# A routed mixture kernel: where the third routing's values are read back, a second PSUM bank, and new places for the routing passes

## The chip, the cores and the metric

One core of one Trainium2 chip. The time is that of one execution on the device, in microseconds (us). The engines are TensorE (PE in the profile: matmuls; its weight loads are PEld), VectorE (DVE), ScalarE (ACT), GpSimd (POOL) and SyncE (SP, which here only starts transfers).

## The reference

Three stages, one after the other. `x` has 1792 rows of 768. The second stage has 8 experts, each of which takes 224 tokens; who goes where is decided by a greedy walk over all logits in falling order.

```python
# 1. sigmoid attention, 4 x 12 heads, 448 tokens, head size 64
scores = scale * np.matmul(q, k.transpose(0, 1, 3, 2)) - np.log(S)
x = np.matmul(1.0 / (1.0 + np.exp(-scores)), v)        # -> (1792, 768)
# 2. routed experts: each token to one expert, each expert full at 224
logits = x @ w_gate
for idx in np.argsort(-logits.flatten()):
    tok, e = idx // E, idx % E
    if assigned[tok] >= 0 or counts[e] >= cap: continue
    assigned[tok] = e; counts[e] += 1
h = np.maximum(x[mask] @ w1[e], 0.0); out[mask] = h @ w2[e]
# 3. a common network with PReLU, d_ff = 2048
h = x @ w_in
g = np.maximum(h, 0.0) + alpha * np.minimum(h, 0.0)
return g @ w_out
```

## The kernel before

**The routed part.** The greedy walk is done as eight routings (r = 0 to 7; "the third" is r = 2). Each finds, for the experts still open, the threshold of the 224th largest value, picks the one expert that is settled by it and its tokens, and closes both. `rank(r)` finds the threshold in eight **passes**: in each, VectorE compares all values (`rank_in`, 128 x 1792) with a trial value and counts the hits, then a few tiny operations make the next trial. For that each expert's 1792 values must stand on 16 partitions. From the third routing on they get there through DRAM: `store_suit` writes `suit` to `suit_flat` (56 KB), `spread_suit` reads it back 16 times over into `rank_in` (896 KB). Both are issued by GpSimd, in one queue with its gathers. `fill(r)` then makes the flags of the tokens, their places and their indices, in three parts between which TensorE does small sums (`spread_thr`, `sum_flags`, `sum_idx`), and the next values.

**The big products.** Every product is made of three float32r matmuls (high x high, high x low, low x high); the high part is a rounding by ScalarE and the low part a subtraction by VectorE. A weight chunk so prepared is a **unit**, in a ring of 12 slots. TensorE walks through steps, one unit each, 60 to a pair of experts: the first expert's w1 (steps 0 to 5, `hidden`, L902), its w2 (6 to 13, `returned`, L932), the second expert's w1 (14 to 19) and w2 (20 to 27), then the common network of both for 448 columns (28 to 59): `ffn_in(m)` (L955) at 28, 29, 31, 33 ... makes one of 16 pieces of h, and `ffn_out(m)` (L967) at 30, 32, 34 ... adds its product with w_out into six banks (`OUT_BANK + d`, banks 1 to 6). There are four pairs (`q`, 0 to 3). w1 and w2 chunks are gathered by GpSimd (L567, L575), since the expert is known only when the kernel runs; SyncE loads the common network's units from DRAM (L511), each once its slot is free.

**Between two steps of the common network** ScalarE empties bank 0 (`above`, `below`, L1151 and L1152) and counts `in_taken`; VectorE makes PReLU of it (`below`, L1464); ScalarE rounds it (`g_high`); VectorE makes `g_low` (L1469), and only then can `ffn_out` begin. All `ffn_in` write bank 0.

**What sets the order.** All engines walk the same steps. VectorE's function `go(s)` issues its work of all steps up to s: `y_low` at steps 14 and 28, `h_low` (L1450) at 6 and 20, PReLU, `g_low`, the low parts of the gathered tokens (`x_low`, L1433) and of the weight units up to seven steps ahead (L1441). A table says at which step each routing pass stands: `PASS_AT[r]` for the eight passes, and then the steps of threshold, flags, indices (`THR_AT`, `FLAGS_AT`, `IDX_AT`) and of the six pieces in which the gathered tokens are turned (`SEL_AT`). A pass at step s is issued after `go(s)`, and whatever belongs to step s + 1 stands behind it. VectorE works in order, so a pass delays it all by some 3 us.

## Time and profile before

| | us |
|---|---|
| median of 3 runs | 1041.22 (1040.79 to 1042.23) |
| the profiled execution's own time | 1040.79 |
| its span in the trace | 1039.1 |
| TensorE busy | 998.8 (96%) |
| VectorE, ScalarE, GpSimd busy | 572.7 (55%), 389.3 (37%), 188.0 (18%) |
| granted TensorE clock, mean | 0.992 |

The span is the trace from the first to the last instruction. A busy TensorE says that matmuls were under way, not that they ran at full speed; the clock column (1.00 is 2.4 GHz, 0.50 is 1.2 GHz) tells the latter. Rows of the trace name an instruction by its line, and what ended the idle time before it.

### The profile page before, as it was taken

How to read it: one execution, taken by the hardware profiler on the slowest of the kernel's cores; microseconds unless marked ns; L12 is line 12 of the kernel's file. 1: busy time of each engine (PE TensorE's matmuls, PEld its weight loads, DVE VectorE, ACT ScalarE, POOL GpSimd, SP SyncE). 2: the span in 40 equal slices, each digit the busy share in tenths (PEclk: the TensorE clock that was granted, in tenths of full speed). 3: DMA queues.
4: the chain of work that ended last, by engine and by line, in shares of the span. 5: the costliest groups of instructions: out<-in, count | busy, mean ns of one | idle time of the engine just before them, and what ended most of it. 6: DMA issues, size and time to landing. Idle time of an engine off the chain costs nothing.

```text
span 1039.1 us, 16704 instructions
## 1 busy us (share of the span) xinstructions
PE 998.8 (96%) x6533; PEld 857.1 (82%) x6533; DVE 572.7 (55%) x1299; ACT 389.3 (37%) x625; POOL 188.0 (18%) x202
## 2 busy tenths in 40 slices
PE   8999999988979999999999999999999999999997
PEld 5555555557978898799989998998999999989996
DVE  4444444598655827947953685496439537221112
ACT  5676676401341124356322224542222356122212
POOL 0010100105520011243301015350100335100001
PEclk9999999999989999999999999999999999999999
DMA  9999996407488685866877855679696436976601
GB/s 210 271 274 273 256 287 198 175 21 249 152 278 277 209 224 181 282 142 214 290 282 234 252 172 122 202 217 377 212 237 213 158 113 193 337 263 215 215 27 54
DMA packets 121476, 222.34 MB, mean 214 GB/s; under 512 B 51424, under 2 KB 69216, under 8 KB 121408
## 3 DMA queue, kind: packets, MB, share of 16 engines
q1 hardware_dynamic: 87152, 120.11, 37.3%
q0 software_dynamic: 21280, 91.59, 28.4%
q10 hardware_dynamic: 12976, 9.70, 3.9%
q8 instruction: 47, 0.77, 0.3%
q14 instruction: 21, 0.17, 0.0%
HBM read 184.84 MB, written 36.52 MB: 213 GB/s over the span
## 4 chain that ended last, share of the span: by engine, by line
PE 85%; DVE 9%; issue 2%; ACT 2%; DMA 1%; POOLq 0%; POOL 0%; DVEq 0%; ACTq 0%
PE psum L955 20%; PE psum L967 19%; PE psum L932 11%; PE psum L902 11%; PE psum L694 8%; PE psum L678 7%; DVE hits L1541 4%; PE psum L897 2%; PE psum L662 2%; PE psum L705 1%; PE psum L927 1%; DMA stage<-x_rows,tok_idx 1%; DVE unit L1441 1%; PE psum L849 1%; PE psum L713 1%
## 5 line engine op out<-in xcount | busy, mean ns | idle before, releaser
L955 PE MATMUL psum<-y_high,unit 128*128 128x448 f32 x768 | 230.9, 368 | 4.4 <-ACT below L1152 4.3
L967 PE MATMUL psum<-g_high,unit 128*128 128x448 f32 x756 | 227.8, 369 | 4.3 <-DVE g_low L1469 4.2
L955 PEld LDWEIGHTS psum<-y_high,unit 128*128 128x128 f32 x768 | 144.2, 188 | 17.9 <-ACT below L1152 5.8
L967 PEld LDWEIGHTS psum<-g_high,unit 128*128 128x128 f32 x756 | 142.0, 188 | 18.9 <-DVE g_low L1469 7.8
L955 PE MATMUL psum<-y_low,unit 128*128 128x448 f32 x384 | 140.3, 365 | 0.0
L1441 DVE TENSOR_TENSOR unit<-raw,unit 128x768 fp32r<-128x768 f32 (+1 forms) x106 | 109.9, 1059 | 51.5 <-ACT unit L1125 44.8
L967 PE MATMUL psum<-g_low,unit 128*128 128x448 f32 x378 | 138.2, 366 | 0.0
L1151 ACT ACTIVATE above<-psum 128x448 f32<-128x448 f32 x64 | 34.9, 545 | 248.8 <-PE psum L955 248.8
L932 PE MATMUL psum<-h_high,unit 128*128 128x224 f32 x672 | 118.5, 280 | 8.8 <-issue 8.8
L1464 DVE SCALAR_TENSOR_TENSOR below<-below,neg_alpha,above 128x448 f32<-128x448 f32 x64 | 43.8, 684 | 147.0 <-ACT below L1152 146.8
L902 PE MATMUL psum<-x_high,unit 128*128 128x224 f32 x672 | 117.3, 276 | 0.0
L932 PEld LDWEIGHTS psum<-h_high,unit 128*128 128x128 f32 x672 | 105.5, 196 | 9.4 <-issue 9.3
L1062 ACT ACTIVATE probs<-psum,gate_bias 112x896 f32<-112x896 f32 x96 | 91.5, 1004 | 55.7 <-PE psum L678 55.7
L1125 ACT CAST unit<-raw 128x768 fp32r<-128x768 f32 (+1 forms) x106 | 93.7, 923 | 29.6 <-DMA raw<-in_moe_w_dram,w_idx 29.2
L902 PEld LDWEIGHTS psum<-x_high,unit 128*128 128x128 f32 x672 | 103.7, 192 | 0.1
L1541 DVE TENSOR_SCALAR_CACHE_REDUCE hits<-rank_in,trial 128x1792 bf16<-128x1792 f32 x49 | 101.6, 2073 | 0.0
L932 PE MATMUL psum<-h_low,unit 128*128 128x224 f32 x336 | 93.4, 278 | 0.0
L567 POOL DMA_INDIRECT raw<-in_moe_w_dram,w_idx x48 | 48.9, 1019 | 245.8 <-PE psum L967 142.6
L902 PE MATMUL psum<-x_low,unit 128*128 128x224 f32 x336 | 92.1, 274 | 0.0
L575 POOL DMA_INDIRECT raw<-in_moe_w_dram,w_idx x64 | 71.9, 1123 | 70.5 <-PE psum L902 20.7
L694 PE MATMUL psum<-probs,v_in 112*64 112x448 f32 x384 | 82.5, 551 | 0.0
L955 PEld LDWEIGHTS psum<-y_low,unit 128*128 128x128 f32 x384 | 72.2, 188 | 5.5
(184 smaller groups left out, 1319.4 us busy)
## 6 DMA issues: line engine op xcount, KB each, us to landing
unit<-ffn_parts SPq DMA_DIRECT2D x120, 768.0 KB, 6.7
ffn_parts<-pre_parts POOLq DMA_DIRECT2D x24, 768.0 KB, 6.7
ffn_parts<-unit SPq DMA_DIRECT2D x8, 768.0 KB, 5.5
q_in<-in_q_dram SPq DMA_DIRECT2D x24, 224.0 KB, 5.5
v_in<-in_v_dram SPq DMA_DIRECT2D x24, 224.0 KB, 7.5
x_rows<-x_tok POOLq DMA_DIRECT2D x8, 672.0 KB, 5.9
rank_in<-suit_flat POOLq DMA_DIRECT2D x6, 896.0 KB
k_in<-in_k_dram SPq DMA_DIRECT2D x23, 224.0 KB, 7.0
```

What stands on the lines that cost most here:

```text
L567: pool.indirect_dma_start(out=raw[:, u % UNIT_RING, LOW, :], out_offset=None, in_=w1_rows, in_offset=at(w1_idx[:, r % IDX_RING, c:c + 1])) ...
L575: pool.indirect_dma_start(out=raw[:, u % UNIT_RING, LOW, 0:D], out_offset=None, in_=w2_rows, in_offset=at(w2_idx[:, r % IDX_RING, c:c + 1] ...
L678: last = pe.matmul(psum[0:P, 2 * h + c, 0:S], k_part[hp % 2][rows, j * P:(j + 1) * P], q_part[hp % 2][rows, :], start=(i == 0), stop=(i == 2))
L694: last = pe.matmul(O[DH * h:DH * h + DH, 0:S], v_in[hp % V_RING][:, h, kj, :], probs[hp % 2][:, h, kj, :], start=(kj == 0), stop=(kj == JT ...
L902: last = pe.matmul(to, w, x[r % 2][:, c, :], start=(opens and i == 0), stop=(closes and i == 2), skip_group_check=True)
L932: last = pe.matmul(to, w, h[:, c, :], start=(opens and i == 0), stop=(closes and i == 2), skip_group_check=True)
L955: last = pe.matmul(psum[:, IN_BANK, 0:PAIR], w, y[:, c, :], start=(c == 0 and i == 0), stop=(c == DC - 1 and i == 2))
L967: last = pe.matmul(psum[:, OUT_BANK + d, 0:PAIR], w, g[:, m % 2, :], start=(m == 0 and i == 0), stop=(m == (FC - 1 if q < GROUPS - 1 else ...
L1062: act.activation(probs[hp % 2][:, h, 2 * step:2 * step + 2, :], psum[0:P, 2 * h:2 * h + 2, 0:S], ACT.Sigmoid, bias=gate_bias[:], scale=flo ...
L1125: act.copy(unit[:, u % UNIT_RING, HIGH, 0:width(u)], raw[:, u % UNIT_RING, LOW, 0:width(u)]).then_inc(w_rounded, 1)
L1441: dve.tensor_tensor(unit[:, u % UNIT_RING, LOW, 0:width(u)], raw[:, u % UNIT_RING, LOW, 0:width(u)], unit[:, u % UNIT_RING, HIGH, 0:width( ...
L1541: then(dve.tensor_scalar(marks, values, limit[:].bitcast(F32), None, ALU.is_ge, ALU.add, accum_out=counts[:]))
```

## The change

1. The third routing's store and read are taken from GpSimd's queue and put into SyncE's, ahead of the common network's loads: the store when the values are made, the read when the store has landed and the second expert's tokens are gathered. VectorE's first pass of r = 2 waits for a semaphore of their own.
2. `ffn_in(1)` writes bank 6, the last of the six of the result, instead of bank 0, and no longer waits for bank 0 to be emptied. `ffn_out(0)` waits, before its last product (the one that opens bank 6), for ScalarE to have emptied it.
3. In later even routings two gathers stand between store and read.
4. The passes of r = 2, r = 3 and of the even routings r = 4 and 6 stand at other steps.

```diff
+        def in_bank(m):
+            return OUT_BANK + DC - 1 if m == 1 else IN_BANK
...
                 if r == 2:
-                    passes, later = (21, 22, 23, 29, 30, 31, 32, 33), (34, 35, 37, 41)
+                    passes, later = (21, 22, 23, 24, 29, 30, 31, 32), (33, 34, 36, 40)
                 elif r == 3:
-                    passes, later = range(45, 53), (54, 55, 57, STEPS + 5)
+                    passes, later = (42, 43, 44, 46, 48, 50, 51, 52), (54, 55, 57, STEPS + 5)
                 elif r % 2 == 0:
-                    passes, later = (9, 11, 13, 16, 22, 24, 28, 29), (31, 32, 34, 38)
+                    passes, later = (9, 11, 13, 16, 18, 21, 23, 25), (31, 32, 34, 38)
...
+            sp.wait_ge(suit_done, 3)
+            sp.dma_start(suit_flat[0].rearrange("e (p g) -> p e g", g=G), suit[:]).then_inc(third_stored, 16)
+            sp.wait_ge(third_stored, 16)
+            for t in range(TILES):
+                sp.wait_ge(first_gathered[t], 32)
+            sp.dma_start(rank_in[:], suit_flat[0].unsqueeze(1).to_broadcast([E, DIGIT, P * G])).then_inc(third_loaded, 16)
             for duo in range(GROUPS):
                 for u in range(STEPS * duo + 2 * OWN, STEPS * duo + STEPS):
...
-            store_suit(2)
-            gather_w2(1, range(3))
-            spread_suit(2)
-            gather_w2(1, range(3, EC))
+            gather_w2(1)
...
                     if q < GROUPS - 2:
-                        repeat_suit(2 * q + 4)
-                    gather_w2(2 * q + 2, range(early, EC))
+                        store_suit(2 * q + 4)
+                    gather_w2(2 * q + 2, range(early, min(early + 2, EC)))
+                    if q < GROUPS - 2:
+                        spread_suit(2 * q + 4)
+                    gather_w2(2 * q + 2, range(early + 2, EC))
...
             def ffn_in(q, m):
                 u = in_unit(q, m)
                 routing(u)
-                if m > 0:
+                if m > 1:
                     pe.wait_ge(in_taken, FC * q + m)
...
-                        last = pe.matmul(psum[:, IN_BANK, 0:PAIR], w, y[:, c, :],
+                        last = pe.matmul(psum[:, in_bank(m), 0:PAIR], w, y[:, c, :],
...
+                    if m == 0 and d == DC - 1:
+                        pe.wait_ge(in_taken, FC * q + 2)
...
-                        dve.wait_ge(rank_loaded, 16 * (r - 1))
+                        if r == 2:
+                            dve.wait_ge(third_loaded, 16)
+                        else:
+                            dve.wait_ge(rank_loaded, 16 * (r - 2))
```

What stands in GpSimd's row around the second expert's gathers: before, the third routing's store (`suit_flat`) and read (`rank_in`) among the gathers of w1 (128 x 1024) and w2 (128 x 768), ...

```order
L584 DMA stage<-x_rows,tok_idx 112x768 x2
L567 DMA raw<-in_moe_w_dram,w_idx 128x1024 x3
L607 DMA suit_flat<-suit 112x8x16
L575 DMA raw<-in_moe_w_dram,w_idx 128x768 x3
L611 DMA rank_in<-suit_flat 128x1x1792
L575 DMA raw<-in_moe_w_dram,w_idx 128x768 x5
```

... and now, in the same row, followed by the next pair's tokens and the fourth routing's store and read:

```order
L598 DMA stage<-x_rows,tok_idx 112x768 x2
L581 DMA raw<-in_moe_w_dram,w_idx 128x1024 x3
L589 DMA raw<-in_moe_w_dram,w_idx 128x768 x8
L598 DMA stage<-x_rows,tok_idx 112x768 x2
L621 DMA suit_flat<-suit 112x8x16
L625 DMA rank_in<-suit_flat 128x1x1792
```

The two have gone to SyncE, and the eight w2 gathers are one run.

VectorE's row in the second and the third pair, from the fourth pass of r = 4 and 6 to the low part of h (`hits` begins a pass, and the four rows with it are its rest; `unit` is the split of weight chunks), before:

```order
L1541 TENSOR_SCALAR hits,counts<-rank_in,trial 128x1792
L1542 STREAM_TRANSPOSE spread<-counts 128x32
L1544 SCALAR_TENSOR_TENSOR spread_own,digit<-spread,by_digit 128x32
L1558 TENSOR_TENSOR trial<-digit,base 128x1
L1561 TENSOR_TENSOR base<-trial,next_bits 128x1
L1441 TENSOR_TENSOR unit<-raw,unit 128x768 x3
L1450 SCALAR_TENSOR_TENSOR h_low<-psum,h_high 128x448 x4
L1441 TENSOR_TENSOR unit<-raw,unit 128x768 x2
```

And now, from the end of the fourth pass:

```order
L1580 TENSOR_TENSOR base<-trial,next_bits 128x1
L1457 TENSOR_TENSOR unit<-raw,unit 128x768 x2
L1560 TENSOR_SCALAR hits,counts<-rank_in,trial 128x1792
L1561 STREAM_TRANSPOSE spread<-counts 128x32
L1563 SCALAR_TENSOR_TENSOR spread_own,digit<-spread,by_digit 128x32
L1577 TENSOR_TENSOR trial<-digit,base 128x1
L1580 TENSOR_TENSOR base<-trial,next_bits 128x1
L1457 TENSOR_TENSOR unit<-raw,unit 128x768
L1466 SCALAR_TENSOR_TENSOR h_low<-psum,h_high 128x448 x4
L1457 TENSOR_TENSOR unit<-raw,unit 128x768 x2
```

The fifth pass stands between the second and the third split, ahead of the low part of h.

VectorE's row in the first pair, around the low part of y, now (before, the pass rows that stand first here came behind `y_low` and `below`):

```order
L1560 TENSOR_SCALAR hits,counts<-rank_in,trial 128x1792
L1561 STREAM_TRANSPOSE spread<-counts 128x32
L1563 SCALAR_TENSOR_TENSOR spread_own,digit<-spread,by_digit 128x32
L1577 TENSOR_TENSOR trial<-digit,base 128x1
L1580 TENSOR_TENSOR base<-trial,next_bits 128x1
L1474 TENSOR_TENSOR y_low<-psum,y_high 128x2x224 x3
L1480 SCALAR_TENSOR_TENSOR below<-below,neg_alpha,above 128x448
L1560 TENSOR_SCALAR hits,counts<-rank_in,trial 128x1792
```

One more pass (the fourth) stands ahead of `y_low`; behind `below` follows a pass as before, now the fifth.

## Rows read from the trace of the kernel before

**Rows 1.** The page, part 1: busy us, share of the span, instructions

```profile
PE 998.8 (96%) x6533; PEld 857.1 (82%) x6533; DVE 572.7 (55%) x1299; ACT 389.3 (37%) x625; POOL 188.0 (18%) x202
```

**Rows 2.** Waits (total, times, longest), then the chain (start, us, what)

```profile
PE psum L932 <- issue: 8.8, 3, 7.4
...
300.08 7.38 issue
307.47 19.19 PE psum L932 x144
...
492.94 16.08 PE psum L902 x144
510.21 16.31 PE psum L932 x144
```

**Rows 3.** Timelines of ScalarE and VectorE: start, us, instruction [idle before, releaser]

```profile
305.01 0.83 ACT L1125 CAST unit<-raw 128x768 fp32r<-128x768 f32 x1 [0.82 <-DMA raw<-in_moe_w_dram,w_idx]
...
306.75 2.21 DVE L1450 SCALAR_TENSOR_TENSOR h_low<-psum,h_high 128x448 fp32r<-128x448 f32 x4
...
325.92 1.97 DVE L1458 TENSOR_TENSOR y_low<-psum,y_high 128x448 fp32r<-128x448 f32 x3 [5.43 <-ACT y_high L1146]
```

**Rows 4.** Table by stretches: busy of each engine, clock, DMA share, GB/s

```profile
281.00:290.00 9.00, 9.00 (x74) 8.98 (x75) 7.93 (x11) 7.49 (x12) 6.59 (x7) 1.00 0.91 307
290.00:293.00 3.00, 3.00 (x30) 3.00 (x28) 2.72 (x3) 1.61 (x2) 2.39 (x3) 1.00 0.49 151
293.00:303.30 10.30, 7.08 (x64) 6.90 (x62) 0.66 (x1) 0.83 (x1) 2.75 (x3) 1.00 0.99 294
303.30:307.40 4.10, 0.00 (x0) 0.00 (x0) 2.78 (x5) 3.22 (x6) 0.00 (x0) 0.50 1.03 401
307.40:313.40 6.00, 5.93 (x28) 5.96 (x29) 5.90 (x12) 1.64 (x3) 0.00 (x0) 0.50 0.47 159
```

**Rows 5.** Timelines of GpSimd, SyncE and TensorE around the read

```profile
288.24 0.68 POOL L611 DMA_DIRECT2D rank_in<-suit_flat  x1 [1.19 <-DMA suit_flat<-suit]
289.22 1.64 POOL L575 DMA_INDIRECT raw<-in_moe_w_dram,w_idx  x1 [0.30 <-issue]
...
292.15 39.00 SPq L511 DMA_DIRECT2D unit<-ffn_parts  x13
...
280.93 0.80 PE L791 MATMUL psum<-ident,stage 112*128 112x112 f32 x6 [0.76 <-DMA stage<-x_rows,tok_idx]
```

**Rows 6.** Timeline of VectorE ahead of h_low, second and third pair

```profile
504.02 2.07 DVE L1541 TENSOR_SCALAR_CACHE_REDUCE hits<-rank_in,trial 128x1792 bf16<-128x1792 f32 x1
...
506.89 2.69 DVE L1441 TENSOR_TENSOR unit<-raw,unit 128x768 fp32r<-128x768 f32 x3
509.49 2.21 DVE L1450 SCALAR_TENSOR_TENSOR h_low<-psum,h_high 128x448 fp32r<-128x448 f32 x4
...
701.68 2.21 DVE L1450 SCALAR_TENSOR_TENSOR h_low<-psum,h_high 128x448 fp32r<-128x448 f32 x4
```

**Rows 7.** Waits from 326 to 367 us

```profile
PE psum L808 <- DVE thr_rows L1563: 0.7, 1, 0.7
```

**Rows 8.** VectorE's busy time and TensorE's waits from 396 on, and its idle time earlier

```profile
396.70:447.90 51.20, 49.27 (x120) 1.00 0.71 230
...
PE psum L967 <- DVE g_low L1469: 2.1, 2, 1.2
...
PE psum L814 <- DVE flags L1595: 0.8, 1, 0.8
...
PE psum L808 <- DVE thr_rows L1563: 0.6, 1, 0.6
...
391.05 0.39 DVE L1433 TENSOR_TENSOR x_low<-psum,x_high 128x224 fp32r<-128x224 f32 x1 [2.83 <-ACT x_high L1117]
```

**Rows 9.** Waits for bank 0 in the whole trace, and TensorE's timeline

```profile
PE psum L955 <- ACT below L1152: 4.3, 4, 1.1
...
335.77 0.47 PE L967 MATMUL psum<-g_high,unit 128*128 128x448 f32 x1 [0.21 <-DVE g_low L1469]
...
535.69 0.47 PE L967 MATMUL psum<-g_high,unit 128*128 128x448 f32 x1 [0.28 <-DVE g_low L1469]
```

8 lines of the change are left out of this document (5 added, 3 removed).

## The prediction

> **What bounds the kernel now.** I read the page first, for the busy shares: TensorE works in 998.8 of 1039.1 us [rows 1], so the change can give back only time in which TensorE stands still or runs slowly. Then the list of waits and the chain, for where it stands. The largest wait is "psum L932 <- issue", 8.8 us in three cases, the longest 7.4 [rows 2]. L932 is the product with w2, and the chain shows the first two places: 7.38 us ahead of 307.47, and 1.2 ahead of 510.21; for the third 8.8 leaves 0.2 [rows 2]. "issue" says only that the profile names no releaser. The kernel does: L932 waits for h_low, which VectorE makes in program order behind the splitting of the w2 chunks. At 306.75 it starts h_low, and ScalarE had rounded the sixth chunk, the last one ahead of it, at 305.01, after a wait for that chunk's transfer [rows 3]. So the 7.38 us are a late transfer.
>
> Third, the table by stretches [rows 4]. While TensorE stood, its granted clock fell from 1.00 to 0.50 (1.2 GHz), at 303.3, that is 3.2 us after its last matmul at 300.08, and it stayed there to about 313.4, so 6 us of matmuls ran at half speed. The 144 matmuls took 19.19 us against 16.31 in the next pair [rows 2]: 2.88 us more. The stall costs 7.4 + 2.9 = 10.3 us in all.
>
> Fourth, the transfers. In GpSimd's queue the read of the values (896 KB, issued at 288.24) stands between the third and the fourth w2 chunk (289.22) [rows 5]. From 290 to 293 the DMA engines were busy for 0.49 and moved 151 GB/s, against 307 before and 401 after [rows 4].
>
> **Part 1, SyncE stores and reads the values.** The store leaves as soon as the values are made, the read at about 281, when the second tokens are in (TensorE turned the last of them from 280.93), instead of at 288.24 [rows 5]. The read then shares the engines with three w1 chunks (512 KB) and the w2 chunks (384 KB each), instead of blocking five of the latter. The w1 chunks have some microseconds in hand: TensorE reads one every 2.7 us from 284 to 300. How much earlier does the sixth w2 chunk land? No row shows this mixture, so I bound it. Lower end: the same bytes move at the same rates, and only the half idle stretch 290 to 293 is filled: 3 us x 0.51 = 1.5 us. Upper end: the chunk is never late. TensorE goes on 0.7 us after h_low begins (306.75 and 307.47 [rows 2, 3]); with L932 at 300.3, 0.2 us behind the product before it as in the third case, h_low begins at 299.6, 7.1 us earlier. I take 4.5, near the middle: the queue no longer holds five chunks back, but from about 294 SyncE's FFN loads (first issued at 292.15 [rows 5]) take half of the engines, as before. The gap is then 2.9 us, shorter than the 3.2 after which the clock fell, so the 2.88 us of slow matmuls go too.
>
> The Trainium skill ("DMA: Bandwidth & Descriptors", Issuing engines are not separate DMA queues) says that transfers issued from several engines run on the same 16 DMA engines and interleave, and that only issuing time is saved. By that rule the sum takes the lower end, 1.5 us, here; it speaks against the change and is rival A.
>
> SyncE itself: the FFN loads queue behind its new waits, but the first one left at 292.15, 11 us after the read will have. A VectorE pass needs the values only after 304. Both cost nothing; without that cover each us of a late read would delay the first pass, and so y_low, by one.
>
> **Part 2, passes of the third routing (21,22,23,24,29..32).** The fourth pass moves ahead of y_low. VectorE stood idle there for 5.43 us [rows 3], of which 2.88 belong to the slow clock; 2.55 us remain for a pass of 2.87 (504.02 to 506.89 [rows 6]): 0.3 us late. y_low, and all behind it, is 4.5 + 2.88 - 0.3 = **7.1 us earlier**.
>
> Behind it four passes stand where five stood, but the first still stands between below and g_low, so out(0) starts where it did. The last pass now waits for below(2): in(2) ends at 343.5 on the old clock, ScalarE takes 1.05, below 0.6, pass and threshold 3.1, so it is 348.2, and TensorE is free for step 33 at 347.2. A gap of 1.0 against one of 0.7 at step 34 [rows 7]: **+0.3**.
>
> **Part 3, passes of the fourth routing (42,43,44,46,48,50,51,52).** From 396.7 to 447.9 VectorE was busy for 49.27 of 51.2 us, and TensorE waited there for g_low 2.1, the threshold 0.6 and the flags 0.8 us [rows 8]. In steps 42 to 44 VectorE had idle pieces of 2.8 us in each [rows 8]. Walking through with a pass of 2.87 to 3.06 (3.7 for the first), a split of 0.87, below and g_low of 0.6 each, and 3.8 to 3.95 us for a step: three passes are through when the first began, all g_low are in time, and the flags come at about 433.9 on the old clock instead of 436.7, after a wait of 1.1. **-2.75**.
>
> **Part 4, passes of the fifth and seventh routing (9,11,13,16,18,21,23,25).** This is the part that costs. Before, VectorE had no idle time ahead of h_low at 509.49: the pass, three splits and h_low follow one on the other, and TensorE waited 1.19 us for it; in the third case, at 701.68, it was 0.2 us late [rows 2, 6]. Now a whole pass (step 18) goes ahead of h_low: +2.87 in each of the two, gaps of 4.1 and 3.1 us. What comes back: no pass stands behind y_low any more.
>
> **Part 5, second w_in piece in the result's last bank.** TensorE waited 1.07 us in four places for ScalarE to empty bank 0, 4.3 us together [rows 9]. Now it goes on; it then waits at most for g_low. In pairs 1 and 2 g_low also comes 3 us earlier, so the 0.28 there goes as well [rows 9]: -1.35 each. In the last pair -1.07. In the first pair a pass (332.2 to 335.1) still delays g_low to 335.7, and out(0) starts at 335.77 as before [rows 9]: nothing. The new wait ahead of the sixth product of out(0) is met 2 us early. Parts 4 and 5: 2 x (2.87 - 1.35) - 1.07 = **+2.0**.
>
> **The clock in the 4.1 us gap.** Only one long gap is in the rows, and there the clock fell after 3.2 us. 4.1 is longer, so I count one fall at the price of the one seen, **+2.9**. The GpSimd moves for the even routings cost nothing: the first pass on those values comes long after them, and the two chunks that go ahead wait for freed slots; a late chunk would cost its delay, as in the first pair.
>
> **Sum.** -7.1 + 0.3 - 2.75 + 2.0 + 2.9 = -4.7 us (-4.65). Against the profiled execution's own 1040.79 us (span 1039.1 and 1.7 around it) that is 1036.1; the median of the runs lies 0.4 above that one: **1036.5 us**.
>
> **Rivals.**
> A, *nothing lands much earlier*: the read slows whatever it runs beside, and the chunk gains 1.5 us. For it: 0.99 busy from 293 to 303 [rows 4]. Against: 290 to 293 show that the read alone can't fill the engines. The gap is 5.9 us, the clock falls as before: -1.5 + 0.3 - 2.75 + 2.0 + 2.9 = +0.95, 1042.2 us.
> B, *the clock falls in all three gaps* (2.9, 4.1 and 3.1 us), on the slower side. For it: in the moved passes' gaps TensorE stands nearly as long as 3.2 us. The price of a fall lies between 2.9 and 4.7: the slow stretch seen lasted 10.1 us, and with 0.7 of it idle 9.4 would run at half speed. With 3.8 each: -7.55 + 11.4 = +3.85, 1045.1 us. It decides once the three cost over 7.55 us together, 2.5 each.
> C, *the clock falls nowhere, or the chunks land in time*: -7.55 with the taken landing and -10.1 with the upper end: 1033.7 to 1031.1 us. For it: 4.1 us is not much over 3.2, and only one case was seen.
> D, *the moved passes hide*: if VectorE were ahead before h_low, part 4 would cost nothing: -4.65 - 5.74 = -10.4, 1030.8 us. Against it: one row follows the other without a gap there [rows 6]. I give it little, and count it with C.
>
> **Chances.** Forecast 0.50, A 0.14, B 0.12, C with D 0.24. The range reaches to C's inner half and to A: 1031.5 to 1042. What a measurement can tell from no change is about 0.2%, 2.1 us. Faster takes the forecast and C and little else: 0.74. Same: A and the mild part of B, 0.16. Slower: the rest of B and a part of A, 0.10.
>
> **What would show it.** Right: the read's packets in SyncE's queue between 282 and 293; ScalarE's rounding of the sixth w2 chunk at 299 to 302; L932 starting at 302 to 304 with clock 1.00; waits of 4 and 3 us ahead of the next two L932; no wait of L955 on below; the flags' wait of the fourth routing 2 to 3 us earlier against its step 42. Wrong: a w1 chunk that TensorE waits for before 300 (the read then costs there), a clock of 0.50 around the third pair's gap too (B) or around neither (C), or gaps there without 2.87 us more, which would mean that I misread the order of the passes.

## The result, and the profile after

| | before | after |
|---|---|---|
| median, us | 1041.79 (1039.1 to 1042.9, 7 runs) | 1044.72 (1042.38 to 1045.88, 7 runs) |
| ratio | | 1.0026, 95% interval 1.0014 to 1.0037 |
| profiled execution, us | 1040.79 | 1045.71 |
| its span, us | 1039.1 | 1044.0 |
| TensorE's granted clock, mean | 0.992 | 0.987 |

The changed kernel is 2.7 us slower: a small difference, but the interval of the ratio does not reach 1. The ratios here and below leave out the rare run that lies far above the rest of its kernel (one of h4 with 1114.8 us, and one of the kernel before with 1653.8 us, beside e1, e2 and e3). The forecast was 1036.5, with 1031.5 to 1042 as its range: wrong in sign.

The page, part 1, of the kernel after (busy us, share of the span, instructions):

```profile
PE 1000.8 (96%) x6533; PEld 862.0 (83%) x6533; DVE 573.4 (55%) x1299; ACT 389.3 (37%) x625; POOL 184.6 (18%) x200
```

TensorE's waits after (total, times, longest), and the chain at the three places of [rows 2]:

```profile
PE psum L946 <- issue: 15.8, 3, 8.6
...
PE psum L983 <- DVE g_low L1485: 2.8, 4, 1.5
PE psum L822 <- DVE thr_rows L1582: 2.4, 2, 1.4
PE psum L828 <- DVE flags L1614: 1.7, 2, 1.1
```

```profile
300.84 8.61 issue
309.45 18.62 PE psum L946 x144
...
508.38 4.07 issue
512.46 17.85 PE psum L946 x144
...
704.22 3.12 issue
707.33 19.33 PE psum L946 x144
```

L946 is the w2 product (before L932), L969 and L983 are `ffn_in` and `ffn_out` (L955, L967), L1141 is ScalarE's rounding (L1125), L1466 is h_low (L1450), L1457 the split (L1441) and L1560 the pass (L1541). The waits of L955 on `below` [rows 9] are gone, as forecast. The wait for the late chunk isn't: 8.61 us where 7.38 were. The two gaps in the later pairs are 4.07 and 3.12, as forecast (4.1 and 3.1), but the 144 matmuls behind each took 17.85 and 19.33 us instead of 16.31: the clock fell in both.

SyncE's queue (store, read, first network loads), then ScalarE's rounding of the first and the sixth w2 chunk, after:

```profile
274.96 0.32 SPq L504 DMA_DIRECT2D suit_flat<-suit  x1
281.73 0.75 SPq L508 DMA_DIRECT2D rank_in<-suit_flat  x1
292.83 25.76 SPq L525 DMA_DIRECT2D unit<-ffn_parts  x7
```

```profile
298.44 0.83 ACT L1141 CAST unit<-raw 128x768 fp32r<-128x768 f32 x1 [3.74 <-DMA raw<-in_moe_w_dram,w_idx]
...
306.99 0.83 ACT L1141 CAST unit<-raw 128x768 fp32r<-128x768 f32 x1 [0.65 <-DMA raw<-in_moe_w_dram,w_idx]
```

The read was issued 6.5 us earlier than before (288.24 [rows 5]), at 281.73. The sixth chunk, the one that h_low waits for, came at 306.99 instead of 305.01 [rows 3]; this trace runs 0.76 us behind the other at that place (300.84 against 300.08), so 1.2 us later where I had it 4.5 earlier. (How far this place scatters from trace to trace stands under e1.) The table by stretches says why (stretch, length, busy of PE, PEld, DVE, ACT and POOL, clock, DMA share, GB/s):

```profile
285.00:290.00 5.00, 5.00 (x47) 5.00 (x47) 4.61 (x6) 2.68 (x5) 3.78 (x5) 1.00 0.99 201
290.00:293.00 3.00, 3.00 (x30) 3.00 (x29) 0.00 (x0) 0.00 (x0) 2.32 (x3) 1.00 1.04 214
293.00:299.00 6.00, 6.00 (x56) 6.00 (x55) 1.23 (x1) 1.61 (x2) 0.00 (x0) 1.00 1.01 207
...
304.00:309.45 5.45, 0.00 (x0) 0.03 (x1) 3.69 (x6) 4.05 (x8) 0.00 (x0) 0.51 0.97 377
```

The reader is to compare the last two columns. From 285 to 299 the DMA engines are fully busy and move only 201 to 214 GB/s; five microseconds later, just as busy, they move 377. The half idle stretch of before [rows 4] is filled, but at little more than half of the rate that busy engines reach later. So all that I wanted from the earlier issue was paid for by the transfers beside it.

The same view at the two later gaps:

```profile
509.00:513.00 4.00, 0.55 (x3) 0.58 (x3) 3.86 (x11) 1.42 (x2) 0.00 (x0) 0.91 0.98 390
...
704.00:707.40 3.40, 0.28 (x3) 0.13 (x2) 3.26 (x10) 2.13 (x4) 0.00 (x0) 0.92 1.02 401
```

A mean of 0.91 over 4 us is 0.7 us at half speed, so the clock fell at 512.3; likewise 0.92 over 3.4 us puts the other fall at 706.9. And VectorE ahead of h_low, with the fifth pass between the splits:

```profile
508.00 2.08 DVE L1560 TENSOR_SCALAR_CACHE_REDUCE hits<-rank_in,trial 128x1792 bf16<-128x1792 f32 x1
...
511.74 2.21 DVE L1466 SCALAR_TENSOR_TENSOR h_low<-psum,h_high 128x448 fp32r<-128x448 f32 x4
```

### The profile page after: what moved, and what is told of

It is laid out like the page before. It is cut to its first block, busy times and chain, and to the rows that moved or that the text cites. A ratio compares the mean times of both kernels' runs of the same rounds, so it can differ in the third digit from the quotient of the medians.

```text
span 1044.0 us, 16699 instructions
## 1 busy us (share of the span) xinstructions
PE 1000.8 (96%) x6533; PEld 862.0 (83%) x6533; DVE 573.4 (55%) x1299; ACT 389.3 (37%) x625; POOL 184.6 (18%) x200
## 4 chain that ended last, share of the span: by engine, by line
PE 87%; DVE 5%; DMA 3%; issue 3%; ACT 2%; POOL 0%; POOLq 0%; DVEq 0%; ACTq 0%
PE psum L969 21%; PE psum L983 19%; PE psum L946 12%; PE psum L916 11%; PE psum L708 8%; PE psum L692 6%; DVE hits L1560 2%; PE psum L911 2%; PE psum L676 2%; DMA rank_in<-suit_flat 1%; PE psum L719 1%; PE psum L941 1%; DMA stage<-x_rows,tok_idx 1%; PE psum L863 1%; PE psum L727 1%
## 5 line engine op out<-in xcount | busy, mean ns | idle before, releaser
L983 PE MATMUL psum<-g_high,unit 128*128 128x448 f32 x756 | 227.4, 368 | 3.0 <-DVE g_low L1485 2.8
L969 PE MATMUL psum<-y_high,unit 128*128 128x448 f32 x768 | 229.8, 368 | 0.1
L983 PEld LDWEIGHTS psum<-g_high,unit 128*128 128x128 f32 x756 | 142.0, 188 | 16.2 <-DVE g_low L1485 5.1
L969 PEld LDWEIGHTS psum<-y_high,unit 128*128 128x128 f32 x768 | 144.3, 188 | 12.2 <-issue 0.8
L969 PE MATMUL psum<-y_low,unit 128*128 128x448 f32 x384 | 140.3, 365 | 0.0
L1457 DVE TENSOR_TENSOR unit<-raw,unit 128x768 fp32r<-128x768 f32 (+1 forms) x106 | 110.4, 1060 | 53.1 <-ACT unit L1141 52.7
L983 PE MATMUL psum<-g_low,unit 128*128 128x448 f32 x378 | 138.1, 365 | 0.0
L946 PE MATMUL psum<-h_high,unit 128*128 128x224 f32 x672 | 122.3, 285 | 15.8 <-issue 15.8
L946 PEld LDWEIGHTS psum<-h_high,unit 128*128 128x128 f32 x672 | 108.5, 201 | 16.4 <-issue 16.3
L1141 ACT CAST unit<-raw 128x768 fp32r<-128x768 f32 (+1 forms) x106 | 93.8, 924 | 28.3 <-DMA raw<-in_moe_w_dram,w_idx 28.2
L1560 DVE TENSOR_SCALAR_CACHE_REDUCE hits<-rank_in,trial 128x1792 bf16<-128x1792 f32 x49 | 101.6, 2074 | 0.0
L946 PE MATMUL psum<-h_low,unit 128*128 128x224 f32 x336 | 95.2, 283 | 0.0
L969 PEld LDWEIGHTS psum<-y_low,unit 128*128 128x128 f32 x384 | 72.2, 188 | 5.5
```

Source lines behind the costliest of these rows:

```text
L946: last = pe.matmul(to, w, h[:, c, :], start=(opens and i == 0), stop=(closes and i == 2), skip_group_check=True)
L969: last = pe.matmul(psum[:, in_bank(m), 0:PAIR], w, y[:, c, :], start=(c == 0 and i == 0), stop=(c == DC - 1 and i == 2))
L983: last = pe.matmul(psum[:, OUT_BANK + d, 0:PAIR], w, g[:, m % 2, :], start=(m == 0 and i == 0), stop=(m == (FC - 1 if q < GROUPS - 1 else ...
L1141: act.copy(unit[:, u % UNIT_RING, HIGH, 0:width(u)], raw[:, u % UNIT_RING, LOW, 0:width(u)]).then_inc(w_rounded, 1)
L1457: dve.tensor_tensor(unit[:, u % UNIT_RING, LOW, 0:width(u)], raw[:, u % UNIT_RING, LOW, 0:width(u)], unit[:, u % UNIT_RING, HIGH, 0:width( ...
L1560: then(dve.tensor_scalar(marks, values, limit[:].bitcast(F32), None, ALU.is_ge, ALU.add, accum_out=counts[:]))
```

## The experiments

All ratios are against the kernel before, run on the same chip in the same session; 0.001 is 1.04 us. Runs of different sessions are best compared by their ratios. A slot is the step at which a pass stands.

| experiment | median us (runs) | ratio, 95% interval |
|---|---|---|
| e1 SyncE's read alone | 1041.59 (12) | 0.9997, 0.9985 to 1.0010 |
| e2 changed kernel, even passes of before | 1038.48 (10) | 0.9968, 0.9953 to 0.9982 |
| e3 changed kernel, read on GpSimd | 1044.73 (12) | 1.0028, 1.0016 to 1.0041 |
| f1 read behind all w2 gathers | 1031.69 (5) | 0.9906, 0.9892 to 0.9921 |
| f2 the bank alone | 1039.89 (12) | 0.9987, 0.9977 to 0.9998 |
| f3 read on GpSimd, passes between h_low and y_low | 1034.04 (5) | 0.9932, 0.9919 to 0.9945 |
| g1 changed kernel, four copies | 1036.71 (7) | 0.9948, 0.9929 to 0.9967 |
| g2 g1 and f3's passes | 1025.63 (5) | 0.9844, 0.9820 to 0.9868 |
| g3 f1, third routing behind y_low | 1029.54 (5) | 0.9888, 0.9869 to 0.9907 |
| h1 before, four copies | 1030.73 (4) | 0.9899, 0.9882 to 0.9915 |
| h3 before, two copies | 1031.93 (6) | 0.9908, 0.9883 to 0.9933 |
| h4 before, eight reads | 1037.89 (12) | 0.9954, 0.9939 to 0.9969 |

e4, f4, h2, h5 and h6 only add reads at the end of the kernel before; their own times say nothing.

### First: which part costs, and is it who issues the read?

**e1**, the kernel before with the change's SyncE lines and nothing else:

```diff
+            sp.dma_start(rank_in[:], suit_flat[0].unsqueeze(1).to_broadcast([E, DIGIT, P * G])).then_inc(third_loaded, 16)
...
-            store_suit(2)
-            gather_w2(1, range(3))
-            spread_suit(2)
-            gather_w2(1, range(3, EC))
+            gather_w2(1)
```

> The kernel before with part 1 alone: SyncE stores and reads the third routing's values; bank, passes and all later routings as before. Theory 1 (the read slows whatever runs beside it: from 284 to 298 us the changed kernel moved only some 200 GB/s, with both queues live): the sixth w2 chunk is rounded 1 to 2 us later than before, the first stall is 8 to 9 us instead of 7.4, and the time is 0.5 to 2 us above that of the kernel before. Theory 2 (the read on SyncE is good by itself, as was forecast, and what ate it is one of the other parts): the sixth chunk some 4.5 us earlier, the first stall near 3 us, 7 us faster than before.

No difference (0.9997); neither theory had that. In its trace the DMA engines moved 199 GB/s from 290 to 293 at a share of 0.97, and 206 from 293 to 299. The first stall was 7.07 us, and the product before it took 17.3 us (284.77 to 302.06) instead of 16.1, since it waited for a w1 chunk. The Trainium skill ("DMA: Bandwidth & Descriptors", Issuing engines are not separate DMA queues), by which another issuing engine saves issue time only, agrees with this.

The first stall scatters, and five more traces tell by how much: e4, f4, h2, h5 and h6 are the kernel before up to their last 60 us. With the trace of before, the stall is 7.0 to 10.0 us long there and the slow clock adds 1.5 to 3.1 us to the product behind it, 9.7 to 11.5 together. The longest is e4's:

```profile
300.79 9.96 issue
310.74 17.86 PE psum L950 x144
```

The same sum is 10.9 in the changed kernel (8.61 + 2.31) and 11.1 in e1 (7.07, 2.85 and the 1.2 of the w1 chunk). So a stall 1.2 us longer and a chunk 1.2 us later are within the scatter. What the traces show is that the earlier read brought nothing near 4.5 us.

**e2**, the changed kernel with `(9, 11, 13, 16, 22, 24, 28, 29)` for the even routings again:

> The changed kernel with the passes of the fifth and seventh routing where they were (9,11,13,16,22,24,28,29). Theory 1 (one pass more ahead of h_low costs its 2.87 us twice and each of the two gaps pulls the clock down): gaps ahead of L946 of 1.2 and 0.2 us instead of 4.1 and 3.1, no clock of 0.50 there, while a pass stands again ahead of g_low, 1.35 us twice: -5.7 - 4.5 + 2.7 = 7.5 us faster than the changed kernel. Theory 2 (the clock falls there for another reason, and the pass is nearly hidden): the clock still falls in both places, 0 to 3 us faster.

6.2 us faster than the changed kernel. Its chain in the second pair:

```profile
507.43 1.20 issue
508.63 16.31 PE psum L946 x144
```

The gap is 1.20 again, the third 0.22, and the matmuls behind them take 16.31. In the changed kernel gaps and slow matmuls at these two places cost (4.07 - 1.20) + (3.12 - 0.22) + (17.85 - 16.31) + (19.33 - 16.31) = 10.3 us; 6.2 of it came back. Most of the rest went behind y_low, where passes stand again: the waits for g_low add up to 6.0 us in e2 and to 2.8 in the changed kernel.

**e3**, the changed kernel with store and read among GpSimd's gathers as before:

> The changed kernel with the third routing's store and read back in GpSimd's queue, the read between the third and fourth w2 gather as before; bank and passes stay changed. Theory 1: the sixth w2 chunk 1 to 2 us earlier than in the changed kernel, first stall near 7.4 us, time 0.5 to 2 us below the changed kernel. Theory 2 (the read on SyncE is a gain, hidden by the passes): 3 to 7 us above the changed kernel.

1044.73 against 1044.72, where both theories had a difference: who issues the read, and 6 us earlier or later, makes no difference. From its table and ScalarE's timeline:

```profile
290.00:293.00 3.00, 3.00 (x29) 3.00 (x29) 2.88 (x4) 2.01 (x3) 2.69 (x2) 1.00 0.58 147
293.00:299.00 6.00, 6.00 (x57) 6.00 (x56) 0.40 (x1) 0.00 (x0) 2.99 (x4) 1.00 1.00 174
```

```profile
307.31 0.83 ACT L1135 CAST unit<-raw 128x768 fp32r<-128x768 f32 x1 [0.62 <-DMA raw<-in_moe_w_dram,w_idx]
```

Three chunks come early and the rest late, the sixth at 307.31 where the changed kernel has 306.99. The slow rate is there wherever the read is: 174 GB/s at a full share from 293 to 299.

**e4** reads, at the end of the kernel before, where nothing else loads: the values as the kernel does it (8 rows, each into 16 partitions), then as many bytes from 128 different rows, then the first once more beside two plain loads.

```diff
+                sp.dma_start(rank_in[:], suit_flat[1].unsqueeze(1).to_broadcast([E, DIGIT, P * G])).then_inc(probed, 16)
...
+                    sp.dma_start(rank_in[:], ffn_parts[0:16].rearrange("u (a p) b d -> (u a) (p b d)", a=8)[:, 0:P * G]
```

> The kernel before, with reads added at its end by SyncE, when its last loads have been issued and the engines are nearly idle; their data is not used. First the 16-fold read of 57 KB (896 KB into 128 partitions) alone, then 896 KB from distinct addresses alone in packets of the same 7168 bytes a row, then the 16-fold read together with two plain reads of 672 KB each. Theory 1 (it is the source that is slow: 16 partitions read the same addresses): first read 6 to 9 us, second 3 to 4 us, and the three together over 9 us, at some 200 GB/s. Theory 2 (the rows of 7168 bytes or the queue are slow, whatever the addresses): first and second alike. Theory 3 (the read only suffers from traffic beside it): first and second both 3 to 4 us.

```profile
992.00:998.00 6.00, 6.00 (x32) 5.55 (x31) 1.31 (x2) 1.55 (x3) 0.00 (x0) 1.00 0.51 118
1001.00:1003.00 2.00, 2.00 (x12) 1.85 (x10) 0.41 (x1) 0.98 (x2) 0.00 (x0) 1.00 0.80 330
1006.00:1015.00 9.00, 9.00 (x46) 8.33 (x46) 1.31 (x2) 1.55 (x3) 0.00 (x0) 1.00 1.00 166
```

Alone the kernel's read moves 118 GB/s at a share of 0.51, different rows 330 at 0.80. Beside plain loads all together move 166 GB/s at a share of 1.00: the read slows its neighbours.

The single packets in the traces say the same. In the changed kernel the 7 KB packets of the read (one row of `rank_in` each) took 561 ns in the median, and the 6 KB packets of the weight chunks about 500 ns from 286 to 293 and 245 ns once the read was over, from 300 to 304. I took the cause to be that few rows serve many readers ("the fold").

### Second: take the read away from the chunks

**f1** issues it behind all w2 gathers, on GpSimd. It also moves passes: those of r = 2 and r = 3, since the values come later, and the even routings' late four to slots 22 to 25, as f3 below:

```diff
             store_suit(2)
-            gather_w2(1, range(3))
-            spread_suit(2)
-            gather_w2(1, range(3, EC))
+            gather_w2(1)
+            spread_suit(2)
```

> GpSimd stores the third routing's values, gathers all of the second w_in and w_out pieces' chunks (the six w2 chunks of the second expert among them), and only then issues the read back; the third routing's passes start 8 slots later; the even routings' late four passes all stand between h_low and y_low (slots 22 to 25), so that neither the flags' gap nor the 2.87 us ahead of L946 is theirs; the bank of the second w_in piece is as in the changed kernel. Theory one (a read of the same rows by 16 partitions is slow at its source and drags all that runs beside it to about 200 GB/s): with no such read beside them the w2 chunks land at the full rate, the sixth by about 4 us earlier (before, its rounding came at 305.0, so about 301), hidden's end sets L946, whose first stall falls from 7.4 to 0 to 3 us, TensorE's clock does not fall there, and the kernel takes 1026 to 1033 us. Theory two (the chunks' own gathers, with their short pieces, hold the rate at 200 GB/s or less and the read adds only its bytes): the stall shrinks by the read's own bytes, 0.9 MB at 200 GB/s or 4 us at most, more likely 1 to 3, the clock falls as before, and the time is 1034 to 1038. If the read comes too late for the third routing's passes, a new gap of some us shows at the passes' slots (DVE waits on its load) and the gain is lost.

```profile
290.00:293.00 3.00, 3.00 (x29) 3.00 (x29) 3.00 (x4) 2.40 (x4) 2.39 (x3) 1.00 0.92 291
...
304.00:310.00 6.00, 6.00 (x56) 6.00 (x55) 0.96 (x1) 0.83 (x1) 0.00 (x0) 1.00 1.03 207
```

```profile
295.75 0.84 ACT L1134 CAST unit<-raw 128x768 fp32r<-128x768 f32 x1 [1.07 <-DMA raw<-in_moe_w_dram,w_idx]
```

The sixth chunk is rounded at 295.75, 11 us before the changed kernel, and TensorE passes the place without a stall. 291 GB/s replace 214 from 290 to 293, and the 207 GB/s have moved to where the late read now is. Its time is another matter: f3, which has the even routings' slots of f1 and the read where it was, is only 2.3 us slower (1034.0), since in f1 the read's landing became a new wait:

```profile
PE psum L962 <- DVE y_low L1467: 6.2, 1, 6.2
```

Two passes stood ahead of y_low and the read landed at 315.6. **g3** puts all eight passes behind y_low (and two of the fourth routing's one slot later):

```diff
-                    passes, later = (21, 22, 29, 30, 31, 32, 33, 34), (35, 36, 38, 42)
+                    passes, later = (29, 30, 31, 32, 33, 34, 35, 36), (37, 38, 40, 44)
```

> As the kernel that issues the read only behind all w2 gathers, with the third routing's passes placed anew: all eight behind y_low (slots 29 to 36), the threshold and the rest from slot 37, the fourth routing's passes in slots 45 to 52. The late read landed at 315.5 there, two passes stood ahead of y_low, and the first w_in piece waited 6.2 us for it, with a clock fall of 6.8 us behind. Theory one (the 6.2 us is only the place of the two passes): the gap goes, less 6 to 9 us against 1031.7, so 1023 to 1027 us. Rival (with the passes behind, the third routing's threshold and selection come late, and a gap opens ahead of the next expert's gathers): 1027 to 1034.

The 6.2 us went, but 1029.5 is only 2.1 us better: 2.4 us came back as a wait for g_low behind a pass, with a slow clock after it, and 1.6 ahead of the next tokens' x_low. Its rival was nearer.

**f2**, the second w_in piece's bank alone:

```diff
-                if m > 0:
+                if m > 1:
                     pe.wait_ge(in_taken, FC * q + m)
...
+                    if m == 0 and d == DC - 1:
+                        pe.wait_ge(in_taken, FC * q + 2)
```

> The kernel before with the second w_in piece's sums in the result's last bank, and nothing else of the change. As read in the profiles: four gaps ahead of the FFN's first w_in pieces and the first w_out piece go (about 0.6 to 1.1 us net, most of it the four waits on below that go, less a gap of about 1.4 ahead of the first w_out piece). Theory one (the bank is right and small): 0.3 to 1.5 us faster than before, ratio 0.9985 to 0.9997. Rival (the new wait inside the first w_out piece costs what the old one did): no difference.

The waits for g_low, first in the trace of before, then in f2's:

```profile
PE psum L967 <- DVE g_low L1469: 4.2, 8, 1.2
...
PE psum L972 <- DVE g_low L1474: 8.3, 9, 1.6
```

1.4 us faster, near the edge of what can be told. The wait on `below` (4.3 us) is gone from its trace, but the wait for g_low, 4.2 us in eight places before, is now 8.3 in nine: VectorE, with a pass ahead of g_low, was the next to be late.

**f3**, the four late passes of the even routings together between h_low and y_low, with the read on GpSimd:

```diff
-                    passes, later = (9, 11, 13, 16, 18, 21, 23, 25), (31, 32, 34, 38)
+                    passes, later = (9, 11, 13, 16, 22, 23, 24, 25), (31, 32, 34, 38)
```

> The third routing's read where the kernel before has it, the bank and the third and fourth routings' passes as in the changed kernel, and the even routings' late four passes in slots 22, 23, 24, 25, all behind h_low and ahead of y_low. Theory one (the changed kernel's loss is the even routings' pass ahead of the fourth w2 chunk's h_low, through a gap and the clock that falls at it): no gaps of 4.1 and 3.1 ahead of the hidden step in the later groups, no clock falls there, 1036 to 1039 us as with the even passes of before, or 1 us better by the gap at the flags. Rival (any four passes close together delay y_low instead): gaps of 1 to 3 us ahead of the first w_in piece in both groups, and 1040 to 1043 us.

```profile
PE psum L977 <- DVE g_low L1479: 2.8, 4, 1.5
```

1034.0, better than either theory, and 10.7 us better than e3, from which it differs in these slots alone (10.0 by the ratios, since the two ran in different sessions). The rows at e2 gave 10.3. g_low waits 2.8 us, not 8.3, h_low isn't delayed, and the clock doesn't fall there. By these waits the bank is worth its 4 us only where no pass stands behind y_low; no run has f3's slots with the old bank.

### Third: what is slow about the read

**f4** reads from 8, 16, 32 and 64 different rows, each alone (shown: 8, 16 and 32).

```diff
+            for i, rows in enumerate((8, 16, 32, 64)):
...
+                sp.dma_start(rank_in[:], src.unsqueeze(1).to_broadcast([rows, 128 // rows, P * G])).then_inc(probed, 16)
```

> The kernel before, with four more reads at its end, each alone: 896 KB into the same 128 partitions from 8, 16, 32 and 64 different rows, each row read by 16, 8, 4 and 2 partitions. Theory one (the source is slow because few addresses serve many readers): about 8 us for 8 rows as found before, and less with each doubling of the rows, down to about 3.5 us at 64, which is what 128 different rows took. Theory two (the slow rate is that of a source within one small stretch, or of the form of the transfer, not of the fold): all four take about the same, 8 us or 3.5 us. Theory three (a limit of rows in one bank of the memory): a step between two of them rather than a slope.

```profile
991.00:996.00 5.00, 5.00 (x26) 4.64 (x25) 1.17 (x2) 1.55 (x3) 0.00 (x0) 1.00 0.50 132
1000.00:1003.00 3.00, 3.00 (x17) 2.78 (x16) 0.87 (x2) 1.55 (x3) 0.00 (x0) 1.00 0.92 229
1008.00:1010.00 2.00, 2.00 (x11) 1.87 (x10) 0.68 (x1) 1.25 (x3) 0.00 (x0) 1.00 0.81 331
```

From its first packet to its last each read took 8.0, 4.9, 3.2 and 3.2 us. The time fell with the fold, as the theory said; this misled me for one more round. The rates per busy engine say more. With 16 engines, 132 / (16 x 0.50) = 16.5 GB/s, 229 / (16 x 0.92) = 15.6, 331 / (16 x 0.81) = 25.5: two things change, the share between 8 and 16 rows, and the speed of a packet between 16 and 32.

**g1** uses it in place: SyncE stores four copies, and each is read by 4 partitions.

```diff
-            sp.dma_start(suit_flat[0].rearrange("e (p g) -> p e g", g=G), suit[:]).then_inc(third_stored, 16)
+            for i in range(4):
+                sp.dma_start(suit_copies[:, i].rearrange("e (p g) -> p e g", g=G), suit[:]).then_inc(third_stored, 16)
...
-            sp.dma_start(rank_in[:], suit_flat[0].unsqueeze(1).to_broadcast([E, DIGIT, P * G])).then_inc(third_loaded, 16)
+            sp.dma_start(rank_in[:], suit_copies[:, :].unsqueeze(2).to_broadcast([E, 4, DIGIT // 4, P * G])).then_inc(third_loaded, 16)
```

> The changed kernel with one edit: SyncE stores the third routing's values four times, as four copies side by side, and the read back takes for each group of four partitions its own copy, so that each stored row is read by 4 partitions and not by 16. Bytes into SBUF, queue, engine and place in the queue stay (three more stores of 56 KB, 0.17 MB). Theory one (the 16-fold source is what holds everything beside it at 200 GB/s): alone a 4-fold read took half as long as the 16-fold one, so the w2 chunks land nearly as they do without any read beside them (sixth rounded at 295.8 there) plus the read's 0.9 MB at 350 GB/s, 2.6 us, so at 298 to 300; the hidden step's first stall of 8.6 us falls to 0 to 2 us and the clock does not fall there; the later gaps of 4.1 and 3.1 us with their clock falls stay: 1032 to 1036 us. Theory two (the read's place beside the gathers is what matters, whatever its source: the gathers' short pieces share badly with any second queue): the sixth chunk comes as in the changed kernel, stall 7 to 9 us, 1043 to 1046.

```profile
285.00:290.00 5.00, 5.00 (x47) 5.00 (x46) 4.01 (x6) 2.08 (x4) 3.91 (x4) 1.00 1.01 403
```

403 GB/s at a share of 1.01 where the changed kernel moved 201 at 0.99, with the read still beside the chunks. Its packets took 272 ns, and the chunks' beside them 234, as alone. The first stall is gone, the gaps of 4.1 and 3.1 remain. The median, 1036.7, is 0.7 above what I expected, and its runs lie far apart (1031.6 to 1040.4; the profile is of the fastest); why is left open.

**g2** is g1 with f3's passes, **h1** the kernel before with nothing but SyncE's read and the four copies.

> As the kernel with four copies, and the even routings' late four passes in slots 22 to 25, between h_low and y_low. If both causes of the loss are found (the 16-fold read; the pass ahead of the fourth h_low with the clock fall behind it) the two gains add: 1034.0 as measured with these slots and the old read, less the first stall of 8.9 us and its clock loss of about 2.9, is 1022 to 1026 us. Rival (taking the stall away lets the load of the later pieces become the next wait, as the 6.2 us gap did where the read came late): 1028 to 1033.

> The kernel before, with the third routing's store and read on SyncE (as in the first experiment, which made no difference by itself) and the four copies; bank and passes are those of before. Theory one (the 16-fold source alone makes the first stall): the sixth w2 chunk is rounded before TensorE ends with w1, the first stall of 7.4 us falls to 0 to 1 and the 2.9 us of slow clock behind it go; all else stays: 1042.0 less 9 to 10.3 is 1032 to 1033 us, and as the kernel with copies landed 1 to 4 us above its forecast, up to 1036. Rival (the gain there came from the copies together with the changed kernel's pass ahead of y_low, and here y_low and its passes wait anyway): 1036 to 1041.

g2 takes 1025.6 us, 16.2 less than before, the best of all; its longest wait ahead of the w2 product is 1.2:

```profile
PE psum L948 <- issue: 1.4, 2, 1.2
```

h1 takes 10.5 us less than before, and its trace has no first stall, only those of 1.20 and 0.23 us that the later pairs had before:

```profile
PE psum L939 <- issue: 1.4, 2, 1.2
```

From e1, which gained nothing, it differs in the copies alone. The prediction had priced that stall at 7.4 + 2.9 = 10.3.

The copies changed the fold and also the outermost dimension of the source, the one that the transfer walks through most slowly: 8 rows by 16 repeats before, and now 32 (8 experts by 4 copies, side by side, merge) by 4. **h2** reads (a) 8 rows with the 16 repeats outermost, (b) 128 different rows with 8 outermost, (c) the kernel's form.

```diff
+            sources = (rows[0:8, 0].unsqueeze(0).to_broadcast([16, 8, P * G]),
+                       rows[:, 0:16],
+                       rows[:, 0:1].to_broadcast([8, 16, P * G]))
```

> The kernel before, with three more reads of 896 KB at its end, each alone: (a) 8 rows, each read 16 times, with the 16 repeats outermost; (b) 128 different rows in 8 groups that can't be merged, so that 8 is the outermost dimension; (c) 8 rows with 8 outermost, the form of the kernel's own read. Theory F (the fold: many readers of one row lengthen the packets): (a) has long packets, about 0.5 us, and (b) short ones, 0.27. Theory L (the lanes: an outermost 8 keeps the transfer to 8 engines): (b) has a DMA share of 0.5 while it runs and (a) of 0.9. Both can hold at once; then (c) is the slowest at 8 us, (a) takes 5 to 6 and (b) 5.

```profile
990.00:993.00 3.00, 3.00 (x17) 2.78 (x16) 0.00 (x0) 0.23 (x1) 0.00 (x0) 1.00 0.97 210
998.00:1003.00 5.00, 5.00 (x27) 4.63 (x26) 1.28 (x2) 1.55 (x3) 0.00 (x0) 1.00 0.51 118
1009.00:1014.00 5.00, 5.00 (x26) 4.65 (x25) 0.69 (x2) 0.57 (x1) 0.00 (x0) 1.00 0.51 118
```

(b) is as slow as (c), and no row in it is read twice. (a), with the fold but 16 outermost, has a share of 0.97. **h5** repeats (b) with other distances between the rows, and (f) reads different rows with 16 outermost (shown: e and f); **h6** reads (g) 128 overlapping rows, so that all partitions read the same 15 KB, with 128 outermost, (h) different rows with 32, (i) with 16.

> The kernel before, with three more reads of 896 KB at its end, each alone and each of 128 different rows: (d) 8 outermost, rows 96 KB and groups 1.6 MB apart; (e) 8 outermost, rows and groups side by side, 7 KB apart; (f) the same rows as (e), with 16 outermost. If 8 outermost alone lengthens the packets, (d) and (e) take 8 us at a DMA share of 0.5 with packets of 0.5 us, and (f) 3.5 us. If the 2.25 MB between groups did it in the last probe, (d) and (e) have packets of 0.27 us and take about 4.5 to 5 us at a share of 0.5.

```profile
1001.00:1005.00 4.00, 4.00 (x21) 3.71 (x20) 0.70 (x2) 0.57 (x1) 0.00 (x0) 1.00 0.50 118
1010.00:1013.00 3.00, 3.00 (x17) 2.78 (x16) 0.00 (x0) 0.00 (x0) 0.00 (x0) 1.00 1.03 256
```

```diff
+            for i, rows in enumerate(([[16, 128]], [[5 * n, 32], [n, 4]], [[9 * n, 16], [n, 8]])):
+                source = bass.AP(ffn_parts.tensor, 0, rows + [[1, n]])
```

> The kernel before, with three more reads of 896 KB at its end, each alone: (g) 128 rows that overlap, each 64 bytes behind the last, so that all 128 partitions read the same 15 KB, with 128 outermost; (h) 128 different rows with 32 outermost (32 groups of 4 that can't be merged); (i) 128 different rows with 16 outermost (16 groups of 8). If the outermost dimension alone sets the rate: (g) and (h) have packets of 0.27 us and take about 3.5 us, (i) has 0.5 us and takes 4.5 at a share of 1.0. If many readers of one place are slow as well: (g) takes 5 to 8 us with packets of 0.5 us or more, and (h) is the fast one.

```profile
989.00:990.00 1.00, 1.00 (x7) 0.93 (x6) 0.00 (x0) 0.00 (x0) 0.00 (x0) 1.00 1.00 409
994.00:995.00 1.00, 1.00 (x6) 0.93 (x5) 0.63 (x1) 0.07 (x1) 0.00 (x0) 1.00 1.07 452
999.00:1001.00 2.00, 2.00 (x12) 1.85 (x11) 0.69 (x1) 1.17 (x3) 0.00 (x0) 1.00 1.09 269
```

(g) ends the theory of the fold: 128 readers of one place run at 409 GB/s. What sorts all shapes is the outermost dimension of the source. (f) and (i) took 4.7 and 4.9 us with packets of about 0.5 us; for (f) I had expected 3.5. All thirteen shapes, each 896 KB and alone, GB/s per busy engine being rate / (16 x share):

| outermost | shapes | DMA share | GB/s | per busy engine |
|---|---|---|---|---|
| 8 | 8 rows x 16 repeats; 8 x 16 different rows, near and far | 0.50 to 0.51 | 118 to 132 | 14.5 to 16.5 |
| 16 | 16 repeats x 8; 16 rows x 8 repeats; 16 x 8 different rows | 0.92 to 1.09 | 210 to 269 | 13.5 to 15.6 |
| 32, 64, 128 | 4 repeats; 2 repeats; different rows; overlapping rows | 0.72 to 1.07 | 301 to 452 | 25.5 to 26.4 |

The Trainium skill ("DMA: Bandwidth & Descriptors", Why a DMA increments its semaphore by 16 and not by 1) says that a transfer runs on as many engines, 16 at most, as divide the outermost dimensions of both sides. The shares of 0.5 with 8 outermost agree with that. The step from 15 to 25 GB/s between 16 and 32 outermost is a second one, and these runs show it without its cause. In all thirteen shapes outermost times inner is 128, so the table can't tell "16 or fewer outermost" from "8 or more within". h4 below speaks for the former: its reads have 16 outermost and nothing within, and its packets took 519 ns beside the chunks, where g1's took 272. And slow packets don't come with the form every time: in the trace of before the read's first 79 packets, over 4 us, took about 0.3 us each with 8 outermost, and only then 0.5.

In place, with 16 outermost: **h3** has two copies instead of four, **h4** no copies and eight reads, one for each expert (16 repeats outermost):

```diff
-            sp.dma_start(rank_in[:], suit_flat[0].unsqueeze(1).to_broadcast([E, DIGIT, P * G])).then_inc(third_loaded, 16)
+            for e in range(E):
+                sp.dma_start(rank_in[DIGIT * e:DIGIT * e + DIGIT], suit_flat[0][e:e + 1].to_broadcast([DIGIT, P * G])
+                             ).then_inc(third_loaded, 16)
```

> The kernel before, store and read on SyncE, with two copies: 16 rows, each read by 8 partitions, and 16 outermost. All else as with four copies (1030.7 us). Theory F: packets of the read stay at about 0.5 us, as the 16 rows alone had, and the chunks beside it stay slow; first stall 4 to 8 us, 1036 to 1042. Theory L: the read spreads over 16 engines, the stall goes, 1030 to 1033.

> The kernel before, store and read on SyncE, no copies: the read is issued as eight, one for each expert, each of one row into 16 partitions with 16 outermost. Every row is still read 16 times, now by 16 engines in a short time. Theory F: no better than the single read (1041.6), packets of 0.5 us or longer and a first stall of 6 us or more, 1040 to 1046. Theory L: all 16 engines share it, the stall goes or shrinks to under 2 us, 1030 to 1034.

```profile
285.00:290.00 5.00, 5.00 (x47) 5.00 (x47) 3.38 (x5) 1.46 (x3) 3.78 (x5) 1.00 1.04 232
```

```profile
285.00:290.00 5.00, 5.00 (x46) 5.00 (x45) 4.92 (x6) 3.25 (x6) 3.78 (x5) 1.00 1.03 230
```

The first row is h3's, the second h4's. Both still move 230 GB/s beside the read, as the slow packets say, but for a shorter time: the read's packets run from 283.9 to 291.8 in h3 and from 284.3 to 296.2 in h4, against 284.2 to 299.5 in the changed kernel. h3 keeps a stall of 0.5 us and gains 9.6, h4 one of 3.6 and gains 4.8. Neither theory had h4 right: 16 engines shorten the slow time, they don't end it.

## Why the prediction was wrong

**Part 1 failed, and it alone turned the sign.** Its step "I take 4.5, near the middle" put the sixth chunk 4.5 us earlier; it came 1.2 later. What I missed stood in my own rows: from 290 to 293 the engines were busy for 0.49 and moved 151 GB/s [rows 4], 19 GB/s per busy engine, while 401 at 1.03 is 24. I read the free half as room that the chunks could fill. But it was the sign of a transfer with 8 outermost, and filling it brought 201 to 214 GB/s at a full share, because the read's slow packets also lengthen those beside it (e4: 166 GB/s). Even the lower bound of 1.5 us was no bound: it took the rates to stay as they were. Rival A, that nothing lands earlier and the read slows what runs beside it, had the mechanism; e1 and e3 show the first, e4 and the packets the second, and h1 against e1 that the read's form was the cause. With it the clock fall behind that stall stayed too: 18.62 against 16.31.

In the two traces the w2 product of the first pair ends at 326.66 and 328.07, 1.4 us later; by parts 1 and 2 it was to be about 7 earlier. That is 8.5 of the 9.6 us between forecast (-4.65) and the spans (+4.9). The medians lie only 2.9 apart, so some 2 us of this is the luck of which two executions were profiled; the sign doesn't hang on it.

**The clock, the second miss, +1.7.** "I count one fall at the price of the one seen, +2.9": there were two, at 1.54 and 3.02 us, 4.56 together. The falls came 3.2, 3.9 and 2.6 us after TensorE's last matmul (from 300.84 to 304.1, 508.38 to 512.3, 704.22 to 706.9), so "3.2 us" wasn't a limit under which a gap is safe, and the price of a fall varies by a factor of two, even at one place of one kernel (1.5 to 3.1 us, under e1). Rival B's three falls came true, at 1.5 to 3.0 us each and not 3.8. f3 and e2, without the two longer gaps, have neither fall.

**Part 2's and part 3's gaps** came as worked out: the threshold's wait 1.1 (forecast 1.0), the flags' 1.1 (1.1). From `ffn_out(0)` in the first pair to the gap in the second the kernel after gained 2.1 us (out(0) starts at 337.25 against 335.77, the gap at 508.38 against 509.02); the forecast was 0.3 - 2.75 = -2.45. And "out(0) starts where it did" held: 9.2 us after the w2 product's end (328.07 to 337.25) against 9.1, with a wait for g_low of 1.5 us in the place of 1.07 and 0.21.

**Part 4** was right to a tenth: 4.07 and 3.12 for 4.1 and 3.1. e2 shows that it is the fifth pass in slot 18 (of the four that e2 moves, it alone stood ahead of h_low), f3 that slot 22 costs nothing there.

**Part 5** was right in what goes (four waits of 1.07) and in the two later pairs. That the gain needs the passes moved too is shown by f2, where g_low takes most of it.

Rival D's sum has a slip that changed nothing in the forecast: without the 4.1 us gap the 2.9 for a fall in it goes too, which gives -13.3 and 1027.9 us, not 1030.8.

So parts 3 to 5 held within about one microsecond, the landing failed by 5.7 us in these traces and took the 2.9 of the clock with it, and one more clock fall came.

## What to carry to other kernels

A DMA share near 0.5 with one transfer in flight need not be room for others. Divide the rate by the busy engines, and look at the outermost dimension of the source: here a read with 32 or more outermost, got by storing the 56 KB four times, ended a stall of 10 us, slow clock included, that moving the read to another engine, or 6 us earlier, left as it was. And a pass is best moved into a stretch in which its own engine stands idle and owes nothing, here between h_low and y_low: four passes in slots 22 to 25 instead of 18, 21, 23 and 25 were worth 10 us.

## What the runs showed of the hardware

Two things that I had not expected. A transfer from DRAM to 128 partitions of 7 KB rows, alone, moved 118 to 132 GB/s with 8 outermost, 210 to 269 with 16 and 301 to 452 with 32 or more, whatever its rows were. In the slower two forms single packets took about twice as long (0.5 us against 0.27; 14 to 16 GB/s per busy engine, not 25), as did packets of other transfers beside them (500 ns against 245). Why 16 outermost, which keep all engines busy, have slow packets was not found. And TensorE's clock fell 2.6 us after the last matmul in one gap and 3.9 in another, for 1.5 to 3.0 us of lost time; in e3, in the same two places, it fell 2.1 us after the last matmul (507.62 to 509.74), and 0.4 us after the end of a gap of 3.1 us (707.33 to 707.72).
